# Sharing the first triangular solution between VectorE and GpSimd in a delta-rule and expert kernel

## The reference

```python
for t in range(S):
    y[:, :, t] = einsum('bhd,bhde->bhe', q[:, :, t], state)
    v_old = einsum('bhde,bhd->bhe', state, k_n[:, :, t])      # k_n: keys of unit length
    state = state + beta_t * outer(k_n[:, :, t], v[:, :, t] - v_old)
x = y as (3072, 384)
x = ((x @ w1) * (x @ w2)) @ w3 @ w_out
logits = x @ phi;  d = softmax over tokens;  slot_input = d.T @ x
slot_out = per expert: relu(slot_input @ w1[e]) @ w2[e]
out = softmax over slots(logits) @ slot_out
```

## Time and profile before

| | before |
|---|---|
| median of 3 runs | 493.86 us (493.72 to 497.18) |
| the profiled execution | 495.12 us, of which the span is 493.4 us |
| PE busy | 450.5 us, 91% of the span |
| DVE, ACT, POOL busy | 50%, 46%, 38% |
| HBM traffic | 129 GB/s over the span |
| chain that ended last | PE 71%, DVE 10%, POOL 8%, DMA 5% |

### The profile page before, as it was taken

One profiled execution on the slowest core, in us unless ns is written; L12 is line 12 of the kernel. 1 busy time (PEld: TensorE's weight loads), 2 busy tenths in 40 slices (PEclk: granted clock), 3 DMA queues, 4 the chain that ended last, 5 costly groups with the idle time before them and its releaser, 6 DMA issues.

```text
span 493.4 us, 21402 instructions
## 1 busy us (share of the span) xinstructions
PE 450.5 (91%) x9729; PEld 323.8 (66%) x9729; DVE 244.4 (50%) x499; ACT 227.9 (46%) x408; POOL 188.4 (38%) x329
## 2 busy tenths in 40 slices
PE   4674899998999999999999999999999999999982
PEld 3243467776777777687677777676787777754442
DVE  3899586355553647346284345644362422144123
ACT  1313455553645555655455565554564464224112
POOL 1001499811588403886028880178830000000000
PEclk9965999999999999999999999999999999999997
DMA  8999305320004400054000641000080094699949
GB/s 205 383 243 336 87 3 112 104 49 5 3 19 113 132 5 3 3 131 130 4 3 4 125 116 24 3 4 4 3 337 9 3 356 160 241 418 425 420 169 372
DMA packets 21002, 64.96 MB, mean 132 GB/s; under 512 B 2352, under 2 KB 3760, under 8 KB 20016
## 3 DMA queue, kind: packets, MB, share of 16 engines
q1 hardware_dynamic: 20208, 62.71, 38.7%
q10 hardware_dynamic: 704, 0.89, 0.7%
HBM read 58.87 MB, written 4.72 MB: 129 GB/s over the span
## 4 chain that ended last, share of the span: by engine, by line
PE 71%; DVE 10%; POOL 8%; DMA 5%; issue 3%; SPq 1%; ACT 0%; DVEq 0%; POOLq 0%
PE pA L1201 19%; PE pB L1201 18%; PE pKY L1103 4%; POOL prep_slab L486 4%; DMA step_slab<-e_dram 4%; POOL prod_p L485 4%; PE pD L1137 3%; PE pKY L1152 3%; PE pKY L1118 3%; PE pT L1219 3%; PE pG L1219 3%; PE pD L1227 2%; DVE prep_slab L820 2%; DVE prod_p L819 2%; DMA arena<-kq_dram 2%
## 5 line engine op out<-in xcount | busy, mean ns | idle before, releaser
L485 POOL TENSOR_TENSOR prod_p<-prep_slab 128x30 f32<-128x30 f32 (+9 forms) x150 | 75.4, 502 | 42.4 <-DVE prep_slab L812 31.5
L745 DVE TENSOR_TENSOR arena<-a_sb,pB 128x512 f32<-128x512 f32 x41 | 28.1, 686 | 120.3 <-PE pB L1201 120.2
L486 POOL TENSOR_TENSOR prep_slab<-prep_slab,prod_p 128x30 f32<-128x30 f32 (+9 forms) x150 | 82.4, 549 | 11.8
L524 ACT ACTIVATE step_slab<-pKY 32x384 f32<-32x384 f32 x92 | 44.3, 482 | 32.8 <-PE pKY L1152 31.1
L1201 PE MATMUL pB<-whi,xhi 128*128 128x512 f32 x135 | 55.8, 414 | 0.0
L1201 PE MATMUL pB<-whi,xlo 128*128 128x512 f32 x135 | 53.2, 394 | 0.0
L1201 PE MATMUL pB<-wlo,xhi 128*128 128x512 f32 x135 | 53.2, 394 | 0.0
L1201 PE MATMUL pA<-whi,xhi 128*128 128x512 f32 x135 | 51.4, 436 | 0.0
L1201 PE MATMUL pA<-wlo,xhi 128*128 128x512 f32 x135 | 47.0, 399 | 0.0
L1201 PE MATMUL pA<-whi,xlo 128*128 128x512 f32 x135 | 46.1, 397 | 0.0
L466 POOL TENSOR_TENSOR arena<-arena,nrm 128x1152 f32<-128x1152 f32 (+1 forms) x11 | 21.1, 1914 | 45.7 <-DVE prep_slab L834 45.0
(11 more groups left out here) (284 smaller groups left out, 889.1 us busy)
## 6 DMA issues: line engine op xcount, KB each, us to landing
arena<-e_dram SPq DMA_DIRECT2D x7, 1536.0 KB, 14.6
arena<-kq_dram SPq DMA_DIRECT2D x44, 192.0 KB, 5.6
late_w<-e_dram SPq DMA_DIRECT2D x4, 1536.0 KB, 10.7
arena<-kv_dram SPq DMA_DIRECT2D x6, 768.0 KB, 5.2
arena<-kv_dram SPq DMA_DIRECT2D x24, 192.0 KB, 5.9
arena<-w3t_dram SPq DMA_DIRECT2D x2, 2048.0 KB, 19.2
arena<-w_dram SPq DMA_DIRECT2D x1, 4096.0 KB, 13.9
out_dram<-late_w SPq DMA_DIRECT2D x6, 576.0 KB, 5.4
```

The costliest lines, as they stand in the source:

```text
L485: link(nc.gpsimd.tensor_tensor(pv, a, x, ALU.mult))
L486: link(nc.gpsimd.tensor_tensor(dst, dst, pv, ALU.add))
L524: nc.scalar.activation(xs[quad(b), :], pKY[quad(quarter(g, b) ^ 1), bank(g, b), 0:DM], ACT.Copy).then_inc(y_done, 1)
L745: nc.vector.tensor_tensor(ab_tile(s, p)[:, half * HF:(half + 1) * HF], a_sb[:], up_bank(t, half, 1), ALU.mult).then_inc(ab_done, 1)
```

## The change

There are four edits. First, block 0's solution is shared: DVE keeps columns 0 to 9 of every step, and POOL works on columns 10 to 31 in a place of its own (`x_late`, in the place of `Z`, with the products in `TM[0]`). Both read the factors from `X`. `scale` then has two instructions in place of one, and the second waits for POOL. Second, PE has two unread products in place of three, one of 512 columns and one of 256; the second waits for the first inc of `x_link`. Third, block 1's keys and queries come in eight DMAs with runs of 4 KB, not 2 KB. Fourth, ACT's two roundings of the weights, `w_high(0)` and `w_high(1)`, each stand later: the first behind `x_high(0)`, the second behind `z_out(1)`.

```diff
+FIRST_COLUMNS = 10
 def pool_base(n):
-    return 0 if is_first(n) else (n - 1) * (1 + 2 * (C - 2))
+    return 0 if is_first(n) else 1 + 2 * (C - 2 - FIRST_COLUMNS) + (n - 1) * (1 + 2 * (C - 2))
...
+        x_late = step_slab[:, 2 * DM:2 * DM + C * (C - FIRST_COLUMNS)].rearrange("p (i j) -> p i j", i=C)
+        prod_late = TM[0][:].rearrange("p a b -> p (a b)")
...
-            reload_kq(1, 1)
+            for e in range(2):
+                for c in range(2):
+                    for r in range(2):
+                        sp.dma_start(KQ[1][64 * r:64 * r + D, e, 4 * c:4 * c + 4].rearrange("p h x t -> p (h x t)"),
+                                     kq[1, r].rearrange("d (e c f) -> d e c f", e=2, c=2)[:, e, c]).then_inc(kq_in[1][r], 16)
...
                 if is_first(n):
+                    pool.wait_ge(prep_link, X_LINK - 1)
+                    link = Link(pool, pool_link, 0)
+                    apart(pool, pool_passed)
+                    j0 = FIRST_COLUMNS
+                    link(nc.gpsimd.tensor_tensor(x_late, At[:, :, j0:], sys_s[:, 5].unsqueeze(2).broadcast_to([128, C, C - j0]),
+                                                 ALU.mult))
+                    pool.wait_ge(prep_link, X_LINK)
+                    for k_ in range(j0 + 1, C - 1):
+                        shape = [128, C - 1 - k_, k_ - j0]
+                        pv = prod_late[:, 0:shape[1] * shape[2]].rearrange("p (i j) -> p i j", i=shape[1])
+                        dst = x_late[:, k_ + 1:C, 0:k_ - j0]
+                        link(nc.gpsimd.tensor_tensor(pv, X[:, k_ + 1:C, k_:k_ + 1].broadcast_to(shape),
+                                                     x_late[:, k_:k_ + 1, 0:k_ - j0].broadcast_to(shape), ALU.mult))
+                        link(nc.gpsimd.tensor_tensor(dst, dst, pv, ALU.add))
...
-            w_high(0)
...
                     if g == 1:
-                        w_high(1)
+                        w_high(0)
...
                     if g == 1:
+                        w_high(1)
                         key_merge(g + 1, 0)
...
-                    pv, a, x, dst = update(prod_p, X, k_, 0, k_)
+                    pv, a, x, dst = update(prod_p, X, k_, 0, min(k_, FIRST_COLUMNS))
...
+                if is_first(n):
+                    j0 = FIRST_COLUMNS
+                    nc.vector.tensor_tensor(X[:, :, 0:j0], X[:, :, 0:j0],
+                                            sys_s[:, 4, 0:j0].unsqueeze(1).broadcast_to([128, C, j0]), ALU.mult).then_inc(scaled_own, 1)
+                    dve.wait_ge(scaled_own, 1)
+                    dve.wait_ge(pool_link, pool_base(1))
+                    nc.vector.tensor_tensor(X[:, :, j0:], x_late, sys_s[:, 4, j0:].unsqueeze(1).broadcast_to([128, C, C - j0]),
+                                            ALU.mult).then_inc(x_link, 1)
...
-            for sem_, i in ((r_done, 1), (x_link, 1), (x_link, 2)):
-                pe.wait_ge(sem_, i)
-                mm(pK[:], ident[:], Macc[:, 0:HF], start=True, stop=True)
+            for sem_, cols in ((r_done, HF), (x_link, HF // 2)):
+                pe.wait_ge(sem_, 1)
+                mm(pK[:, 0:cols], ident[:], Macc[:, 0:cols], start=True, stop=True)
```

More of the change, by code:

```diff
@@ L240, in delta_moe_kernel @@
         nrm_done, vp_done, tm_done = sem("nrm_done"), sem("vp_done"), sem("tm_done")
-        x_link = sem("x_link")
+        x_link, scaled_own = sem("x_link"), sem("scaled_own")
         a_ps = sem("a_ps")
@@ L826, in scale @@
             def scale(n):
-                if not is_first(n):
+                xs_ = scaled(n)
+                if is_first(n):
[6 more added lines that the diff above has]
+                                            ALU.mult).then_inc(x_link, 1)
+                else:
                     dve.wait_ge(pool_link, pool_base(n + 1))
-                xs_ = scaled(n)
-                nc.vector.tensor_tensor(xs_, X[:], sys_s[:, 4].unsqueeze(1).broadcast_to([128, C, C]),
-                                        ALU.mult).then_inc(x_link, 1)
+                    nc.vector.tensor_tensor(xs_, X[:], sys_s[:, 4].unsqueeze(1).broadcast_to([128, C, C]),
+                                            ALU.mult).then_inc(x_link, 1)
                 dve.wait_ge(x_link, 2 * n + 1)
```

## The result

The changed kernel takes 500.64 us (median of 6 runs, 498.48 to 503.44), the kernel before 495.02 us on the same chip (6 runs, 493.72 to 498.0). The ratio is 1.0112, with a 95% interval of 1.0062 to 1.0161: slower by 5.6 us, where 1.1 us was forecast. (The forecast of 495.0 us was counted from 493.86 us; from the 495.02 us of these runs it would be 496.1.) The profiled execution takes 500.66 us with a span of 498.9 us, against 495.12 and 493.4 us.

What follows compares the result with a forecast made beforehand. PE, 91% busy, bounds it, with PE and POOL paths meeting near 101 us. PE path -1.85 + 0.5 + 2.4 = +1.05 us, POOL path +1.0 us; the larger, +1.1 us, gives 495.0 us for 493.86, range 490.9 to 499.2 us.

Steps and rivals of the forecast that it cites:

- The POOL path: DVE's set-up of block 1, POOL's solution, DVE's scaling, then PE's turn at 101.04 us; forecast +1.0 us.
- the clock term: In chunk 0's `solve_rows`, small matmuls run while PE's clock rises from half; forecast +0.5 us.
- If it rises as before: Condition at `solve_rows`: PE's clock rises within 49.5 to 50.0 us as before, so `solve_rows` loses 0.5 us.
- the clock never rises: Rival: PE's clock stays half until the first `up`'s wide products; +4.4 us on the PE path, 498.2 us, chance 0.22.
- The gain of 1.85 us: Shorter unread products let `solve_rows` start at about 48.95 in place of 50.80 us: -1.85 us on the PE path.
- if the fetch stays as late: Condition on PE's stop in the Gram products: they still end at 46.22 us, the unread products at 48.5 us.
- the sum: PE path up to 101 us: -1.85 + 0.5 + 2.4 = +1.05 us; POOL path +1.0 us.
- the last clause of a rival: If the 2.4 us gap at chunk 1 lowers the clock as well, 1 to 2 us more, 500 us; chance 0.06.
- The two paths: PE path and POOL path end together near 101 us; a gain on one alone is worth at most 0.1 us.
- the larger shift: Behind 101 us the kernel moves by the larger of both paths' shifts; forecast +1.1 us.
- PE path: From chunk 0's `solve_rows` at 50.80 us to PE's last work before the turn, 100.95 us; forecast +1.05 us.
- a shift there stays what it is: Behind 101 us PE is busy nearly throughout, so a shift keeps its size to the end.

Runs made afterwards that it cites:

- `only_sharing`: The kernel before with only the first solution shared between DVE and POOL; 496.25 us, ratio 1.0001.
- `only_products`: The kernel before with only the unread products changed, two (512 and 256 columns) for three; 497.55 us, ratio 1.0025.
- `only_roundings`: The kernel before with only ACT's two roundings of the weights moved later; 500.5 us, ratio 1.0086.
- `gap_two_full_unshared`: `gap_two_full` without the sharing and the 4 KB runs; 495.23 us, ratio to the kernel before 1.002.
- `split_at_16`: `gap_two_full` with DVE keeping 16 columns and POOL 16 in the first solution; 496.12 us, ratio to the kernel before 1.001.
- `changed_rounding_in_gap`: The changed kernel with `w_high(1)` moved into ACT's idle time, between `a_out` of chunk 0 and `z_out(1)`; 496.83 us, ratio to the kernel before 1.0028.
- `changed_gap_three`: The changed kernel with `w_high(1)` in ACT's idle time and three full unread products again; 495.3 us, ratio to the kernel before 1.0006.
- `changed_three_products`: The changed kernel with three full unread products again; 499.87 us, ratio to the kernel before 1.0085.
- `gap_two_full`: The changed kernel with `w_high(1)` in ACT's idle time and two unread products of 512 columns; 496.14 us, ratio to the kernel before 1.0022.
- `no_pool_steps`: `gap_two_full` without POOL's 40 instructions in the first solution; 496.89 us, ratio to the kernel before 1.004.

## Why the prediction was wrong

**The sharing** was right in kind and size. The two engines fall into step: 22.28 us measured from DVE's first product to its last sum, 22.75 forecast (21.95 to 44.7); `TM` is ready at 49.08 us, 48.4 with the 0.66 us of the later start taken off, for 48.9. The POOL path came 1 us later, as forecast, shown by `only_sharing`. The rule that I weighed there (the Trainium skill, "SBUF — State Buffer", section "SBUF: two separate sides": a lock for the whole instruction) gave an end near 53 us by the prediction's estimate; the trace does not agree, since DVE ended at 44.89 us. Only part of each instruction kept the other out here.

**The products: the step that failed is the clock term**, "If it rises as before", with +0.5 us. It priced only a late rise, and put a later fall at nothing. The clock rose, and the first 45 matmuls of `solve_rows` lost 0.47 us (1.17 for the 0.70 that they take at full clock in `only_products`), but it fell again at 55 us, within the pauses of chunk 0, and the first `up` ran at half: 5.49 us for 2.84. I had this as a rival by another way (the clock never rises) with a price of the right size. The gain of 1.85 us failed as well. The Gram products ended at 47.21 us and not at 46.22, so "if the fetch stays as late" did not hold in this execution, and the unread products took 2.9 us, not 2.3. So `solve_rows` started 0.73 us earlier and not 1.85. What I had not priced at all is the second stop of PE in "issue", 0.79 us in the changed kernel and 1.70 in `only_products`, inside `solve_rows`. An earlier start runs into it, so nothing of the gain arrived: the first `up` starts 0.75 us late. In all, the sum had -1.35 us for this edit (-1.85 + 0.5), and the runs show +1.1 to +1.3.

**The runs of 4 KB** did nothing that can be told, as forecast: ratio 1.0012 with an interval around 1.

**The roundings** cost PE the 2.4 us that the sum has (2.22 us of idle time measured). The sum lacked the half clock behind the gap, 1.5 us more, which stood only in the last clause of a rival with a chance of .06. `only_roundings` shows that this fall needs no other edit, and so should have been weighed by itself. This is the second step that failed: the mechanism was right, and the term mis-sized, 4.3 us alone and 3.8 to 4.2 us in the other comparisons, for 2.4. That the last clause names 500 us and the median is 500.64 us is in part luck: it supposes a clock that does not rise before the first `up`, where it rose and fell again, and it knows nothing of the 2 us that came back behind 101 us.

**The two paths**: the forecast took the larger shift, 1.1 us. Measured are 7.6 us on the PE path at 108 us, of which some 2 come back. So "a shift there stays what it is" failed as well, in the kernel's favour. That the larger shift decides held: `gap_two_full_unshared` gained 2.2 us on the PE path and nothing at 101 us.

**What stays open.** What decides whether the clock falls at 54 to 55 us: profiles of the same PE program show both. Runs of one kernel scatter by 2 to 7 us, in part more than the two falls cost, and a run without a profile has only its mean clock, not the place of a fall. In `split_at_16` the four executions of 492.5 to 494.1 us have a mean of 0.980 or 0.981 and the other seven, from 494.7 us up, 0.974 or less; in `changed_rounding_in_gap` time and clock do not go together. Nor is it shown why a wait of 2.45 us left the clock full, or that the "issue" stops are late fetches of instructions. No kernel here beats the one before: `changed_gap_three` (1.0006) and `split_at_16` (1.001) cannot be told from it.

## What to carry to other kernels

Before a step is moved in an engine's queue, look for that engine's own idle time and put the step inside it: 2.75 us of rounding were free between two waits of ACT and cost 4 us eight microseconds later, where ACT was full and PE waited for it. Add to such a gap on TensorE what the clock may take behind it (1.5 to 3.1 us here), and to any removed filler what the clock may lose behind it (2.65 us in the first `up`). Before an engine's work is brought forward, look for the next thing that it meets: here a second stop, and at 101 us the other path. This chain of short instructions gained nothing from a second elementwise engine, since both read two operands from SBUF.

## What the runs showed of the hardware

- A gap of 2.2 us on a PE that had run at full clock for over 10 us was followed by half clock in all three kernels with this gap that are profiled: for 3.4 us in the changed kernel and `only_roundings`, for 6.8 us in `changed_three_products`. Of the waits near 101 us, 1.76 us (`gap_two_full`) was followed by 3.4 us at half clock, 1.56 us (`only_sharing`) and 2.45 us (`gap_two_full_unshared`) were not. So a gap of this size can lower the clock and need not.
- DVE and GpSimd, each in a chain of instructions with two SBUF inputs, end in step: DVE's 60 instructions took 22.3 us with GpSimd's 40 beside them and 19.8 us without.
- While DMA moved some 180 to 415 GB/s, PE stood 5.0 to 7.6 us in "issue" among the Gram products, in all 14 profiles. In seven of them it stood again, for 0.2 to 1.7 us, behind the 45th matmul of `solve_rows`, and this second stop ended 6.1 to 6.3 us behind the first. In the other seven `solve_rows` began at 50.64 us or later, or ran at half clock (`no_pool_steps`, from 49.62 us), and no second stop of 0.2 us or more shows.
- Runs of 4 KB in place of 2 KB did not bring the transfers into 48 partitions nearer to the 387 GB/s that w3 has the earlier trace rows: in the changed kernel the queue still moved 207 to 262 GB/s at 28 to 40 us.
